# Attention and two expert layers on one core: a block product ahead of the last turned reciprocals, block sums moved between GpSimd, VectorE and ScalarE, and a shorter wide path

## The reference

```
keep   = (key < n_sink) or (0 <= query - key < window)       # 4 sinks, window 128
a      = softmax(where(keep, q @ k.T / 8, -1e9));  x = a @ v  # per head
g, val = x @ w_gate, x @ w_val                                # 512 -> 1536
x      = (g * sigmoid(g) * val) @ w_out                       # 1536 -> 512
do     = x @ w_skip > 0                                       # top-1 of 8 experts
out    = x + gate * relu(x @ w1[e]) @ w2[e]   where do, else x
```

## Time and profile before

| | |
|---|---|
| Median of three runs | 542.96 us |
| Profiled execution | 542.63 us, span 540.8 us |
| PE busy | 519.2 us, 96% of the span |
| PEld, DVE, ACT, POOL busy | 461.7, 317.7, 215.5, 208.6 us |
| Mean granted TensorE clock | 0.988 of full speed |
| The chain that ended last | 88% on PE |

### The profile page before, as it was taken

One profiled execution on the slowest core, in us unless ns is written; L12 is line 12 of the kernel. 1 busy time (PEld: TensorE's weight loads), 2 busy tenths in 40 slices (PEclk: granted clock), 3 DMA queues, 4 the chain that ended last, 5 costly groups with the idle time before them and its releaser, 6 DMA issues.

```text
span 540.8 us, 11863 instructions
## 1 busy us (share of the span) xinstructions
PE 519.2 (96%) x3889; PEld 461.7 (85%) x3889; DVE 317.7 (59%) x788; ACT 215.5 (40%) x531; POOL 208.6 (39%) x302
## 2 busy tenths in 40 slices
PE   7999996999999999999989999999999999999993
PEld 5777775999999999999968888888988888888882
DVE  6777777877777777777762443733371515451450
ACT  5778762344333333333543424422330313331440
POOL 7255798965656565654600010011121111111111
PEclk9999998899999999999999999999999999999997
DMA  8997530088777777775663111772346855981511
GB/s 229 296 262 208 168 104 4 1 252 252 240 237 224 234 228 244 237 243 154 230 241 129 55 43 58 251 284 86 108 161 240 309 221 173 341 349 32 185 30 29
DMA packets 42470, 99.69 MB, mean 184 GB/s; under 512 B 2736, under 2 KB 15024, under 8 KB 38336
## 3 DMA queue, kind: packets, MB, share of 16 engines
q1 hardware_dynamic: 24784, 61.24, 32.9%
q10 hardware_dynamic: 15088, 29.87, 18.3%
q0 software_dynamic: 2560, 8.09, 4.5%
HBM read 61.11 MB, written 38.07 MB: 183 GB/s over the span
## 4 chain that ended last, share of the span: by engine, by line
PE 88%; DVE 4%; DMA 2%; ACT 2%; issue 2%; POOL 1%; DVEq 0%; ACTq 0%; POOLq 0%
PE bank L1720 13%; PE bank L1538 11%; PE bank L1540 11%; PE bank L1542 10%; PE bank L1650 6%; PE bank L1654 6%; PE bank L1652 6%; PE bank L1526 4%; PE bank L1735 3%; PE bank L1737 3%; PE bank L1736 3%; PE bank L1503 3%; PE bank L1482 3%; DMA xg<-expert_rows 2%; PE bank L1670 2%
## 5 line engine op out<-in xcount | busy, mean ns | idle before, releaser
L1538 PE MATMUL bank<-x_blocks,w_blocks 128*128 128x384 f32 x336 | 113.7, 338 | 3.5 <-issue 2.5
L1540 PE MATMUL bank<-x_blocks,w_blocks 128*128 128x384 f32 x336 | 113.2, 337 | 0.0
L1542 PE MATMUL bank<-x_blocks,w_blocks 128*128 128x384 f32 x336 | 113.2, 337 | 0.0
L1720 PEld LDWEIGHTS bank<-xgT,w_sb 128*128 128x128 f32 x704 | 80.4, 192 | 1.9 <-issue 0.8
L1720 PE MATMUL bank<-xgT,w_sb 128*128 128x96 f32 x704 | 80.7, 275 | 0.7 <-ACT xgT L990 0.7
L1538 PEld LDWEIGHTS bank<-x_blocks,w_blocks 128*128 128x128 f32 x336 | 63.8, 190 | 4.3 <-issue 4.3
L1540 PEld LDWEIGHTS bank<-x_blocks,w_blocks 128*128 128x128 f32 x336 | 63.9, 190 | 0.0
L1542 PEld LDWEIGHTS bank<-x_blocks,w_blocks 128*128 128x128 f32 x336 | 63.8, 190 | 0.0
L1650 PE MATMUL bank<-wo_split,hh_hi 128*128 128x512 f32 x132 | 53.7, 407 | 0.9 <-issue 0.9
L642 POOL TENSOR_TENSOR w_blocks<-w_sum,w_blocks 128x256 fp32r<-128x256 f32 x48 | 36.3, 757 | 44.6 <-ACT w_blocks L803 44.6
L736 POOL DMA_INDIRECT expert_rows<-x,row_i x12 | 11.9, 992 | 107.2 <-DVE row_i L1339 99.5
(11 more groups left out here) (197 smaller groups left out, 953.5 us busy)
## 6 DMA issues: line engine op xcount, KB each, us to landing
expert_rows<-pad ACTq DMA_DIRECT2D x10, 2891.2 KB, 14.6
w_raw<-w SPq DMA_DIRECT2D x16, 1024.0 KB, 7.1
w_sb<-w SPq DMA_DIRECT2D x16, 1024.0 KB, 8.0
w_raw<-w_gv SPq DMA_DIRECT2D x12, 512.0 KB, 10.5
va_sb<-v_long SPq DMA_DIRECT2D x10, 512.0 KB, 4.0
vb_sb<-v_tail SPq DMA_DIRECT2D x10, 320.0 KB, 6.4
k_sb<-kT SPq DMA_DIRECT2D x12, 256.0 KB, 6.1
wo_raw<-w_out SPq DMA_DIRECT2D x4, 768.0 KB, 6.2
```

Source lines behind the costliest of these rows:

```text
L1538: nc.tensor.matmul(ps, wb[:, p, 0, k, :], xb[:, X_OF[p], 0, k, cols], start=(k == 0 and p in (P1, P6, P5, P7)), stop=False, skip_group_che ...
L1540: nc.tensor.matmul(ps, wb[:, p, 0, k, :], xb[:, X_OF[p], 1, k, cols], start=False, stop=False, skip_group_check=True)
L1542: last = nc.tensor.matmul(ps, wb[:, p, 1, k, :], xb[:, X_OF[p], 0, k, cols], start=False, stop=(k == KD // 2 - 1), skip_group_check=True)
L1720: last = nc.tensor.matmul(ps, w1_sb[u][:, k, fc], xgT[:, k * ET:k * ET + ET], start=(k == 0), stop=(k == KD - 1))
```

## The change

The edits are these:

- In the list of steps there is a new kind, C: ScalarE casts the four sums of tile 6, 7 and 8 behind step V of the second pair of tiles 7, 8 and 9, and those of tile 9 ahead of the last R. combine_x has no cast any more; it raises x_summed with the last sum, and xT_ready with A22's lo part. combine_x is not run for tile 10.
- The sums of tiles 10 and 11 are VectorE's, in two functions, first_sums (S1, S2, right behind X) and last_sums (S3, S4; for tile 10 behind the last Q). GpSimd casts the results of tile 10.
- split_s of half 0 for S2 and S1 stands behind the last Q, and for half 1 only S2 stands ahead of the branch; S1 half 1 and S3 in both halves are behind it, S3 half 1 after the first mix. MIXES has v half 0 ahead of m0 half 1.
- TensorE does P1 half 0 ahead of the last R, and P1 half 1 and P6 half 0 ahead of the branch.
- The weight blocks of slice 0 are split three, three and one behind tiles 4, 5 and 6.
- On TensorE the wide path is written with loops over heads and query tiles in place of written-out ones.

```
-W_SPLITS = {4: (0, 1), 5: (2, 3), 6: (4,), 7: (5,), 8: (6,)}
+W_SPLITS = {4: (0, 1, 2), 5: (3, 4, 5), 6: (6,)}
...
                 if hp == HP - 1:
+                    if tile == NT - 1:
+                        steps.append(("C", NT - 3, None, NT - 3 - QT))
                     steps.append(("R", tile, None, psum_use))
...
                 if tile in W_SPLITS and hp == 1:
                     steps += [("W", tile, None, b) for b in W_SPLITS[tile]]
+                if QT < tile < NT - 2 and hp == 1:
+                    steps.append(("C", tile - 1, None, tile - 1 - QT))
...
@@ combine_x (GpSimd)
-                nc.gpsimd.tensor_tensor(s4, a12, s2, ALU.subtract).then_inc(x_step, 1)
-                pool.wait_ge(x_step, t * 4 + 4)
-                nc.gpsimd.tensor_copy(xb[:, S2:S4 + 1, 0, :, at_tok], xr[:, S2:S4 + 1, 1, :, at_tok]
-                                      ).then_inc(xT_ready, 1)
+                nc.gpsimd.tensor_tensor(s4, a12, s2, ALU.subtract).then_inc(x_summed, 1)
...
@@ ScalarE
+                elif kind == "C":
+                    a.wait_ge(x_summed, n + 1)
+                    at_tok = slice(n * P, n * P + P)
+                    nc.scalar.activation(xb[:, S2:S4 + 1, 0, :, at_tok], xr[:, S2:S4 + 1, 1, :, at_tok], ACT.Copy
+                                         ).then_inc(s_hi_made, 1)
...
@@ VectorE
+            def first_sums(tile, made):
+                a21, a22, a11, a12, s1, s2, s3, s4 = parts(tile)
+                then(nc.vector.tensor_tensor(s1, a21, a22, ALU.add))
+                nc.vector.tensor_tensor(s2, s1, a11, ALU.subtract).then_inc(made, 1)
+            def last_sums(tile, made):
+                a21, a22, a11, a12, s1, s2, s3, s4 = parts(tile)
+                nc.vector.tensor_tensor(s3, a11, a21, ALU.subtract).then_inc(made, 1)
+                d.wait_ge(made, 1)
+                nc.vector.tensor_tensor(s4, a12, s2, ALU.subtract).then_inc(made, 1)
...
                     nc.vector.reciprocal(rsum[:, tile % 2, :], rsum[:, tile % 2, :]).then_inc(rsum_ready, 1)
+                    if tile == NT - 1:
+                        last_sums(NT - 2, s_next_to_last)
+                        d.wait_ge(s_hi_made, QT // 2)
+                        split_s(S2, 0)
+                        split_s(S1, 0)
...
+                        if tile >= NT - 2:
+                            d.wait_ge(o_ready, tile + 1)
+                            first_sums(tile, s_next_to_last if tile == NT - 2 else s_last)
...
@@ TensorE
-            for one in ORDER:
-                step(*one)
-            pe.wait_ge(max_ready, NT * H)
-            for j in range(2):
-                wait_for_x(P1, j)
-                next_product(0, P1, j)
+            for kind, tile, h, n in ORDER:
+                if kind == "R" and tile == NT - 1:
+                    pe.wait_ge(max_ready, NT * H)
+                    wait_for_x(P1, 0)
+                    next_product(0, P1, 0)
+                step(kind, tile, h, n)
+            for p, j in PRODUCTS[1:3]:
+                wait_for_x(p, j)
+                next_product(0, p, j)
             with if_wide(pe):
```

More of the change, by code:

```diff
@@ L1064, in _, with parts @@
             then(nc.vector.tensor_scalar(mask[:, 2, 0:P], keep[:, 3, 0:P], -MASKED, MASKED, ALU.mult, ALU.add))
+            def parts(tile):
+                at_tok = slice((tile - QT) * P, (tile - QT) * P + P)
+                return ([raw_x(tile % 2, half) for half in range(2)] + [x0_raw[:, 0:2, at_tok], x0_raw[:, 2:4, at_tok]]
+                        + [xr[:, n, 1, :, at_tok] for n in (S1, S2, S3, S4)])
+            def first_sums(tile, made):
[7 more added lines that the diff above has]
+                nc.vector.tensor_tensor(s4, a12, s2, ALU.subtract).then_inc(made, 1)
             def split_s(n, j):
@@ L1116, in _ @@
                                                 ).then_inc(o_ready, 1)
[L1117 to L1130, removed]
+                        if tile >= NT - 2:
+                            d.wait_ge(o_ready, tile + 1)
+                            first_sums(tile, s_next_to_last if tile == NT - 2 else s_last)
+            last_sums(NT - 1, s_last)
             d.wait_ge(s_last, 3)
[L1132 removed]
+            d.wait_ge(s_hi_made, NT // 2 - 2)
+            d.wait_ge(s_hi_next_to_last, 1)
             d.wait_ge(s2_hi_last, 1)
             split_s(S2, 1)
[L1135 to L1137 removed]
             with if_wide(d):
                 d.wait_ge(a22_lo_last, 1)
+                d.wait_ge(s_hi_last, 1)
                 d.wait_ge(s4_split, 2)
@@ L1278, in split_wo @@
                                             ).then_inc(wo_by_dve, 1)
-            with d.Fori(0, FT1 - 1) as f:
+            d.wait_ge(s_hi_last, 1)
+            split_s(S1, 1)
+            split_s(S3, 0)
+            for name, j in MIXES:
+                mix(0, name, j)
+                if (name, j) == ("u2", 0):
+                    split_s(S3, 1)
+            with d.Fori(1, FT1 - 1) as f:
                 for name, j in MIXES:
@@ new lines, in _ @@
+                    with pe.Fori(0, H) as h:
+                        with pe.Fori(0, QT) as qt:
+                            i = (b * H + h) * QT + qt
+                            pe.wait_ge(all_q_ready, i + 1)
+                            pe.wait_ge(all_o_ready, i + 1)
+                            hold(pe, "pe")
+                            for ps, keys in ((bank[0], slice(0, 512)), (bank[1], slice(512, S))):
+                                last = nc.tensor.matmul(ps[:, 0:keys.stop - keys.start], all_qt,
+                                                        all_k[:, keys], start=True, stop=True)
+                            last.then_inc(all_scores, 1)
+                            pe.wait_ge(all_probs, i + 1)
+                            for t in range(QT):
+                                last = nc.tensor.transpose(bank[2 + t // 4][:, t % 4 * P:t % 4 * P + P],
+                                                           all_p[:, t * P:t * P + P], ident[:, :])
+                            last.then_inc(all_turned, 1)
+                            pe.wait_ge(all_pT_ready, i + 1)
+                            for t in range(QT):
+                                last = nc.tensor.matmul(bank[4][:, 0:D], all_pT[:, t * P:t * P + P], all_v[:, t, :],
+                                                        start=(t == 0), stop=(t == QT - 1))
+                            last.then_inc(all_pv, 1)
@@ L1614, in _ @@
                         for k in range(KD):
-                            last = nc.tensor.transpose(bank[5][:, k * P:k * P + P], all_o[:, qt, k * P:k * P + P],
-                                                       ident[:, :])
+                            last = nc.tensor.transpose(bank[5][:, k * P:k * P + P],
+                                                       all_o[:, qt, k * P:k * P + P], ident[:, :])
                         last.then_inc(all_x_turned, 1)
@@ L1620, in _ @@
                 product(P1, 0)
-                product(P1, 1).then_inc(all_redone, 1)
-            for p, j in PRODUCTS[2:]:
+                product(P1, 1)
+                product(P6, 0).then_inc(all_redone, 1)
+            for p, j in PRODUCTS[3:]:
                 wait_for_x(p, j)
```

70 lines of the change are left out of this document (33 added, 37 removed).

## The result

| | before | after |
|---|---|---|
| median, us | 542.69 (542.26 to 544.45, 4 runs) | 549.99 (548.67 to 551.34, 4 runs) |
| ratio, 95% interval | | 1.0119 (1.01 to 1.0139) |
| profiled execution, us | 542.63 | 548.67 |
| its span, us, and mean granted clock | 540.8 | 547.0, clock 0.985 |

The changed kernel is 1.2% slower: 7.3 us by the medians, 6.04 us between the two profiled executions (that of after is the fastest of its four). The forecast was 549.0.

The account below looks back on a forecast made before the run. TensorE was taken to bound the kernel almost everywhere, the passage being the only thin stage. 7.5 + 0.5 + 0 - 2.85 + 0.85 = +6.0 us gave 548.6 profiled, 549.0 on the median; range 545.3 to 552.5.

Parts of the forecast that it names:

- Part 1: Attention: casts moved from GpSimd to ScalarE wait for GpSimd's sums and hold up the exponentials, +7.5 us.
- the first stall: Attention: ScalarE's first moved cast waits until 63.0, so turned reciprocals come late and TensorE is 2.75 us late.
- the loop: Attention: a chain through four engines takes 9.09 us against a tile of 6.73, 4.7 us for tiles 8 and 9.
- Two signs: Attention: ScalarE idles 3.4 to 4 us before three casts; TensorE idles 2.4 to 2.8 us three times.
- Rival (a): Attention: sums come before ScalarE arrives, so the cast doesn't hold it up; 541.0 us, not slower; chance 0.06.
- rival (b): Attention: the stall comes once and tiles then keep 6.73 us; +1.0 us, 544.0; chance 0.10.
- The clock in attention: Attention: TensorE's new pauses may bring half clock; +0.5 us taken, +3 at most.
- rival (c): Attention pauses bring half clock each time, +3 instead of +0.5, passage at its bound; 552 to 553 us; chance 0.18.
- Part 2: Attention: weight blocks split earlier, behind tiles 4 and 5, fall into pauses; 0, bounds -0.2 to +0.5 us.
- Part 3: Passage from attention to block products: P2 starts at 91.6 against 94.45, -2.85 us, bounds -3.5 to 0.
- Half clock behind P2: Passage: the longer pause brings half clock again for P2 and what follows; +0.85 us, bounds 0 and +1.7.
- just suffices: Passage: splits moved behind VectorE's branch come in time for the products that want them; 0, up to +1 us.

Follow-up runs that it names:

- Experiment 2: The kernel before with only the casts of tiles 6 to 8 moved to ScalarE, at the change's place with its wait: 551.27 us, ratio 1.013.
- experiment 1: The changed kernel with ScalarE's casts of tiles 6, 7 and 8 one tile later in its queue: 541.88 us, ratio 0.9965 against the kernel before.
- experiment 3: The changed kernel with TensorE's wide path written out again over heads and query tiles: 549.42 us, ratio 1.0109 against the kernel before.
- Experiments 6: The kernel of experiment 1 with ScalarE's two P1 copies of slice 0 ahead of its last casts and branch: 541.3 us, ratio 0.9955.
- 7: The kernel with later casts and early P1 copies, with TensorE's wide path written out again: 541.52 us, ratio 0.9965 against the kernel before.
- experiment 5: The kernel of experiment 1 with VectorE's split S1 of half 0 moved behind the last tile's sums: 541.12 us, ratio 0.9961.
- experiment 8: Later casts, early P1 copies, S1 half 0 split behind the last sums, S1 half 1 and S3 half 0 ahead of VectorE's branch: 541.11 us, ratio 0.9948.

## Why the prediction was right

The sum in the prediction was 7.5 + 0.5 + 0 - 2.85 + 0.85 = +6.0 us. The profiled execution took 6.04 more. The mechanism and the two large terms hold. That the last digits agree is luck, twice over: attention with its clock term came out 0.93 us under the sum and the passage 0.15 under it, the half clock 0.2 over it, and 1.1 us were not in the sum at all; and the profiled execution is the fastest of four. By the medians the change costs 7.3 us, by the ratio 6.5.

**Part 1, the first stall and the loop: held.** Predicted: the cast starts at 63.0, TensorE is 2.75 us late, a tile then takes 9.09 us. Measured: 62.90, 2.45 us of idle time, and 8.92 us. The 4.7 us of the loop came out as 2 x (8.92 - 6.73) = 4.4. Two signs were off: ScalarE's idle time was 3.85, 3.29 and 3.30 us for 3.4 to 4, and TensorE's three pauses were not all 2.4 to 2.8 but 2.45, 0.52 and 1.98. With the clock the prediction had 8.0 us and attention is 7.07 us longer. Experiment 2 shows that this edit alone does it, experiment 1 that it is the wait and not the work. Rival (a), that the cast would not hold ScalarE, and rival (b), that the stall would come once, are out by the rows of the three casts.

**The clock in attention: the size was less than I took, and the sign I gave for it was wrong.** I took +0.5 with +3 as the bound, and wrote that a granted clock of 0.5 between 60 and 90 us would mean rival (c), 552 to 553. The clock was 0.5 from 67 to 70 us and the time was not that: one drop is not a drop at every pause. Of three pauses one brought half clock, and the next pause took it up, as the prediction said it would in part: it shrank to 0.52 us, so the cost is nearly nothing. Experiment 2 is a small case of rival (c): half clock behind the last pause, with nothing to absorb it, costs about 1.1 us (8.2 against 7.1).

**Part 2, the weight splits: no sign of them.** Experiment 1 has them where the change puts them, and its tiles take 6.73 us.

**Part 3, the passage: held.** Predicted -2.85 us at P2, measured 4.07 - 7.07 = -3.00. The 0.85 us that the small reciprocal step had lost came back too (0.16 us for 1.01), as experiment 2 shows by itself; the sum had it in the 0.46 us of that step. In experiment 1, without the stall, P2 starts at 92.36 less 0.9, which is 91.46, against 91.6 predicted. The branch lies inside the wait for ScalarE's copy, as the prediction had it, and experiment 3 confirms that the shorter code is worth nothing there. The Trainium skill, "Runtime: NRT & Kernel Launch", section "Instruction fetch mechanics", says that a taken branch stalls when its target lies beyond the fetched pages; the prediction couldn't separate that from the 2.53 us. Experiments 6 and 7 do: 2.67 us with long code, none with short. That fits the rule, though no row shows the fetch itself.

**Half clock behind P2: mis-sized.** I took +0.85 in the middle of 0 and +1.7. The matmuls at half clock ran 5.6 us after and 3.35 before, and half of the difference is +1.1. Counted over matmuls, the 60th row of TensorE from P2 on starts 13.08 us after it, against 12.04 before: +1.04.

**What the sum left out: +1.1 us later.** The last block product of the first expert layer starts 5.1 us late. Then the wait for wo_split is 0.3 longer (1.48 against 1.15), a gap of 0.3 is new just ahead of it, and the wait for the gathered rows xg is 0.4 longer (1.15 against 0.73): 6.2 in the end, the difference of the spans. Experiment 1 has all three as well (1.5 and 1.2 us in its waits), so they don't come from the stall. Experiment 2 has the longer wait for xg but not the one for wo_split. Why they grow was not tried and stays open. The traces narrow it down: the wait for wo_split is 1.43 to 1.48 us in all eight kernels that have the change's MIXES, and 1.15 and 1.13 in the two that have the old one (before and experiment 2). The wait for xg is 0.73 us before, 0.8 in experiment 5 and 1.2 to 1.7 in the others, one profile each, so a part of its growth may be scatter. The two waits and the gap also explain most of why experiment 1 gains 1.9 us and not the 3.0 of its passage: its last product still starts 2.7 us earlier than before.

**A pause of VectorE that I had not seen.** VectorE stands 2.88 us at its own branch in the changed kernel too:

```profile
97.22 0.96 DVE L1104 TENSOR_TENSOR x_blocks<-x_raw,x_blocks 128x768 fp32r<-128x768 f32 x1
101.06 3.61 DVE L1104 TENSOR_TENSOR x_blocks<-x_raw,x_blocks 128x768 fp32r<-128x768 f32 x2 [2.88 <-issue]
```

Before, the stretch between its 0.96 us split and the next two held 0.72 us that the trace puts down to a wait for GpSimd's cast (94.82). It costs nothing in the changed kernel, since TensorE is at half clock and late itself. In experiment 6 it stands between TensorE's waits for splits, which the prediction's "just suffices" did not see. It was not the bound by itself, as experiment 8 took it away and gained nothing that can be measured.

## What to carry to other kernels

Work moved to an engine with room still carries its wait with it, and an in-order queue makes everything behind it wait as well. Ask when the releaser comes and when the engine gets there; here they were 3.3 to 3.9 us apart, and one tile of distance, with not an instruction less, turned 1.2% slower into 0.4% faster. A pause that ends in front of a branch may have two reasons at once, and shortening the code there shows only once the wait beside it is gone. Even then it moved no more than the pause here: in the total the next wait took it up.

## What the runs showed of the hardware

- At the branch TensorE paused 2.67 us with the long wide path behind it and not visibly with the short one (experiments 7 and 6), VectorE 2.88 us in both the changed kernel and experiment 6 (3.33 in experiment 7), and ScalarE 0.92 us (idle on issue ahead of its copy at 97.89 in the changed kernel).
- What was seen of VectorE's pause at its branch depended on the work queued ahead of it: 2.88 us behind one split of 0.96, 1.34 behind two of 2.46 (experiment 5), none behind four of 6.37 (experiment 8). In the first two cases split and pause together are 3.8 us.
- Pauses of nearly one length had unlike ends: 1.98 us left the granted clock at 1.00, 2.03 us in the same place was followed by 0.50. A price for the clock in such a place can only be a range.
- Behind a stretch at half clock the pause was shorter by about what that stretch had lost, as another engine's chain set the period: 0.52 us between pauses of 2.45 and 1.98 (0.49 between 2.50 and 2.03 in experiment 2), with ScalarE's casts 8.9 us apart each time.
